# VectorE takes the narrow expert variant first and computes the output places behind the branch; the last MLP outputs go by token part

## The reference

```python
# attention: B=2, H=8, S=576, D=64, causal window of 128, bias by head
attn = softmax(where(mask, q @ k.T / 8 + bias, -1e9));  x = attn @ v      # 1152 tokens x 512

# top-1 MoE: N=1152 tokens, E=8 experts, D=512, F=1024, capacity = N // E * 2 = 288
expert_idx = argmax(x @ w_gate);  gate_w = softmax(x @ w_gate)[expert_idx]
disp[e, slot] = x[i]                      # a token past its expert's capacity is dropped
y = relu(disp @ w1) @ w2;  out[i] = gate_w[i] * y[expert_idx[i], pos[i]]  # 0 if dropped

# MLP: 1152 x 512 -> 2048 -> 512
h = out @ w_in;  result = (h * sigmoid(h)) @ w_out
```

## Time and profile before

| what | us |
|---|---|
| median of 3 runs | 481.11 |
| lowest, highest | 479.75, 485.68 |
| the profiled execution | 479.0 |
| its span, first to last instruction | 477.3 |
| TensorE busy in it | 445.4 (93%) |
| mean granted TensorE clock | 0.975 |

### The profile page before, as it was taken

How to read it: one execution, slowest core, us unless ns; L and a number is a source line. 1 busy time by engine, 2 the same in 40 slices (tenths; PEclk the granted TensorE clock), 3 DMA queues, 4 the chain that set the end, 5 groups by cost and what they waited for, 6 DMA issues and landing times.

```text
span 477.3 us, 8177 instructions
## 1 busy us (share of the span) xinstructions
PE 445.4 (93%) x2917; PEld 406.8 (85%) x2917; DVE 239.7 (50%) x705; ACT 225.7 (47%) x549; POOL 235.5 (49%) x161
## 2 busy tenths in 40 slices
PE   5899989927999999999999999999999999999992
PEld 4677777727999999999999989998999999999982
DVE  4477888874674866857758442122222222222230
ACT  4777768633585656666566644222222222212221
POOL 3006777742879999899898975820200002000002
PEclk9999999956999999999999999999999999999998
DMA  9999940139858777787577600000100000000001
GB/s 182 277 278 291 290 122 12 46 110 320 300 191 276 280 245 227 228 281 274 201 250 253 237 16 1 1 2 0 67 0 0 0 0 32 34 0 0 0 0 66
DMA packets 54566, 64.28 MB, mean 135 GB/s; under 512 B 32096, under 2 KB 32096, under 8 KB 54528
## 3 DMA queue, kind: packets, MB, share of 16 engines
q1 hardware_dynamic: 52752, 59.08, 39.6%
q0 software_dynamic: 1776, 4.73, 2.7%
HBM read 54.35 MB, written 9.44 MB: 134 GB/s over the span
## 4 chain that ended last, share of the span: by engine, by line
PE 84%; DVE 6%; ACT 4%; issue 3%; DMA 1%; POOL 1%; DVEq 0%; POOLq 0%
PE bank L1151 17%; PE bank L1129 14%; PE bank L1130 14%; PE bank L1131 14%; PE bank L1150 8%; PE bank L1003 4%; PE bank L1148 3%; PE bank L1043 3%; PE bank L1020 2%; PE bank L987 2%; PE bank L1149 2%; ACT prob L548 1%; PE bank L1135 1%; DVE prob L724 1%; DVE x_tile L755 1%
## 5 line engine op out<-in xcount | busy, mean ns | idle before, releaser
L439 POOL TENSOR_TENSOR w_lo<-w_raw,w_hi 128x1024 fp32r<-128x1024 f32 x72 | 178.4, 2500 | 39.5 <-ACT w_hi L578 34.8
L959 DVE TENSOR_TENSOR g_full<-bank,sigmoid 128x384 f32<-128x384 f32 x48 | 26.8, 558 | 135.4 <-ACT sigmoid L666 131.6
L666 ACT ACTIVATE sigmoid<-bank 128x384 f32<-128x384 f32 x48 | 23.6, 492 | 132.7 <-PE bank L1131 124.5
L519 POOL DMA_INDIRECT out_dram<-out_stage,permcol x9 | 8.8, 975 | 150.5 <-DVE out_stage L978 148.6
L578 ACT ACTIVATE w_hi<-w_raw 128x1024 fp32r<-128x1024 f32 x74 | 77.7, 1051 | 0.0
L898 DVE TENSOR_REDUCE bank<-bank 128x192 f32<-128x384 f32 x96 | 53.5, 558 | 43.1 <-PE bank L1151 43.0
L1151 PE MATMUL bank<-hidden,w_hi 128*128 128x384 f32 x224 | 67.0, 362 | 0.0
L1129 PE MATMUL bank<-x_hi,w_hi 128*128 x192 | 65.0, 339 | 0.0
L1131 PE MATMUL bank<-x_hi,w_lo 128*128 x192 | 64.6, 336 | 0.0
L1130 PE MATMUL bank<-x_lo,w_hi 128*128 x192 | 64.4, 336 | 0.0
L1151 PE MATMUL bank<-xT,w_hi 128*128 128x384 f32 x192 | 61.2, 366 | 0.0
(11 more groups left out here) (129 smaller groups left out, 792.5 us busy)
## 6 DMA issues: line engine op xcount, KB each, us to landing
w_raw<-in_moe_w_dram SPq DMA_DIRECT2D x64, 512.0 KB, 5.7
dispatch_dram<-zeros SPq DMA_DIRECT2D x4, 1152.0 KB, 7.8
w_raw<-in_moe_w_in_dram SPq DMA_DIRECT2D x8, 512.0 KB, 4.5
w_raw<-in_moe_w_out_dram SPq DMA_DIRECT2D x8, 512.0 KB, 6.7
dispatched<-dispatch_dram SPq DMA_DIRECT2D x9, 384.0 KB, 7.7
q_raw<-in_q_dram SPq DMA_DIRECT2D x8, 256.0 KB, 5.6
k_raw<-in_k_dram SPq DMA_DIRECT2D x8, 256.0 KB, 6.1
v_raw<-in_v_dram SPq DMA_DIRECT2D x8, 256.0 KB, 5.9
```

What stands on the lines that cost most here:

```text
L439: nc.gpsimd.tensor_tensor(wlo[s][:, sl], raw[s][:, sl], whi[s][:, sl], ALU.subtract).then_inc(pool_lo, 1)
L666: nc.scalar.activation(sig[:, f % 2, :], bank[f % 4][:, 0:TB], ACT.Sigmoid).then_inc(sig_ready, 1)
L959: nc.vector.tensor_tensor(gf[:, f % 2, :], bank[f % 4][:, 0:TB], sig[:, f % 2, :], ALU.mult).then_inc(gf_ready, 1)
```

## The change

- VectorE's branch compares the other way round, so that the narrow variant stands first in its code and the wide one behind it. TensorE and ScalarE branch as before.
- The output places are a function that VectorE calls inside the branch, behind the four `x_low` of expert 0. The copy to `permcol` that ended them is gone; `routed` is told by the instruction before it. The wide variant waits for `routed` in addition.
- SyncE does not wait for `routed` any more. GpSimd waits for `offs_ready` ahead of one subtraction and for `routed` ahead of `tell_places`.
- In each MLP block the outputs of the last four chunks (12 to 15) are taken out of the order and done at the end, by token part: all of part 0, then 1, then 2, except that (part 1, chunk 12) comes ahead of (part 0, chunk 15).

```diff
-        def by_top_count(eng, experts):
+        def by_top_count(eng, experts, narrow_first=False):
 
             n = eng.value_load(top[0:1, 0:1], min_val=0, max_val=C)
-            with eng.If(n > NARROW):
-                experts(C)
+            with eng.If(n <= NARROW if narrow_first else n > NARROW):
+                experts(NARROW if narrow_first else C)
             with eng.Else():
-                experts(NARROW)
+                experts(C if narrow_first else NARROW)
...
             load_dispatched(0)
             sp.wait_ge(xd_in, 16)
 
-            sp.wait_ge(routed, 1)
             load_w1(1, 2)
...
+            pool.wait_ge(offs_ready, 2)
             low_here(1, EARLY - PIECES, EARLY + 1)
...
                 low_here(2 + n // PIECES, n % PIECES, split_by(E, 2 * PIECES + n + 1))
+            pool.wait_ge(routed, 1)
             for t in range(NTOK):
                 tell_places(t)
...
-            link(nc.vector.tensor_scalar(pos8[:], pos8[:], -float(C), 0.0, ALU.add, ALU.max))
...
-            link(nc.vector.tensor_copy(target[:], osum[:]))
-            nc.vector.tensor_copy(permcol[:], target[:, 0:TS]).then_inc(routed, 1)
+            def output_places():
+
+                link(nc.vector.tensor_scalar(pos8[:], pos8[:], -float(C), 0.0, ALU.add, ALU.max))
...
+                nc.vector.tensor_copy(target[:], osum[:]).then_inc(routed, 1)
...
+            linked = chain[0]
+
             def experts(w):
+                chain[0] = linked
                 for c in range(KC):
                     dve.wait_ge(step_done, c + 1)
                     dve.wait_ge(hi_ready, c + 1)
                     x_low(c, bank[c], w)
+                output_places()
                 if w > NARROW:
+                    dve.wait_ge(routed, 1)
                     dve.wait_ge(scattered, 16 * NTOK)
...
             dve.wait_ge(offs_ready, 2)
-            by_top_count(dve, experts)
+            by_top_count(dve, experts, narrow_first=True)
...
+            def last_outputs(tb):
+
+                assert TS == 3
+                f0, last_f = F2C - FQ, F2C - 1
+                turns = [(0, f) for f in range(f0, last_f)] + [(1, f0), (0, last_f)]
+                turns += [(1, f) for f in range(f0 + 1, F2C)] + [(2, f) for f in range(f0, F2C)]
+                for t, f in turns:
+                    if t == 0:
+                        pe.wait_ge(glo_ready, tb * F2C + f + 1)
+                    last = output_part(tb, f, t)
+                    if f == last_f:
                         last.then_inc(o_done, 1)
 
             with pe.Fori(0, NB) as tb:
                 for f in range(F2C + 2):
                     if f < F2C:
                         hidden(tb, f)
-                    if f >= 2:
+                    if 2 <= f < F2C - FQ + 2:
                         output(tb, f - 2)
+                last_outputs(tb)
```

More of the change, by code:

```diff
@@ L878, in _ @@
             nc.vector.tensor_copy(offs[:], off8[:]).then_inc(offs_ready, 1)
-            link(nc.vector.tensor_scalar(pos8[:], pos8[:], -float(C), 0.0, ALU.add, ALU.max))
[L881 to L889, removed]
-            link(nc.vector.tensor_copy(target[:], osum[:]))
-            nc.vector.tensor_copy(permcol[:], target[:, 0:TS]).then_inc(routed, 1)
+            def output_places():
+                link(nc.vector.tensor_scalar(pos8[:], pos8[:], -float(C), 0.0, ALU.add, ALU.max))
+                nc.vector.reduce_sum(droprank[:], pos8[:], axis=AX.X)
+                link(nc.vector.tensor_tensor(oo[:], onehot[:], off8[:].unsqueeze(1).broadcast_to([P, NTOK, E]), ALU.mult))
+                link(nc.vector.reduce_sum(osum[:], oo[:], axis=AX.X))
+                link(nc.vector.tensor_tensor(osum[:], osum[:], place[:], ALU.add))
+                link(nc.vector.tensor_scalar(dtot[:], droprank[:], incl8[:, E - 1:E], None, ALU.add))
+                link(nc.vector.tensor_scalar(keep[:], place[:], float(C), None, ALU.is_lt))
+                link(nc.vector.tensor_tensor(osum[:], osum[:], dtot[:], ALU.subtract))
+                link(nc.vector.tensor_tensor(osum[:], osum[:], keep[:], ALU.mult))
+                link(nc.vector.tensor_tensor(osum[:], osum[:], dtot[:], ALU.add))
+                nc.vector.tensor_copy(target[:], osum[:]).then_inc(routed, 1)
             def take_sum(bk, w):
@@ L1214, in hidden, with output_part @@
                 last.then_inc(h2_done, 1)
+            def output_part(tb, f, t):
+                s, fq = f // FQ, f % FQ
+                row = slice(W_IN + fq * DM, W_IN + (fq + 1) * DM)
+                col = slice(t * P, (t + 1) * P)
+                return triple(bank[4 + t][:], ((ghi[:, f % 4, col], glo[:, f % 4, col]), (whi[s][:, row], wlo[s][:, row])),
+                              f == 0, f == F2C - 1)
             def output(tb, f):
-                s, fq = f // FQ, f % FQ
                 pe.wait_ge(glo_ready, tb * F2C + f + 1)
@@ L1222, in output @@
                     pe.wait_ge(o_dve, tb + 1)
-                row = slice(W_IN + fq * DM, W_IN + (fq + 1) * DM)
                 for t in range(TS):
[L1225 to L1228, removed]
+                    output_part(tb, f, t)
+            def last_outputs(tb):
[8 more added lines that the diff above has]
+                    if f == last_f:
                         last.then_inc(o_done, 1)
```

## The result

The change made the kernel slower, by 0.9%: the median is 484.47 us (480.65 to 490.70) against 480.31 us (476.00 to 486.41), ratio 1.009, 95% interval 1.0066 to 1.0113. The forecast was 476.6 us, in a range of 473.5 to 480.5.

The account below looks back on a forecast made before the run. TensorE was taken as the bound (busy 93% of the span), so only its waits could give time. Gains of 3.3 us at the experts' start and 1.2 at the tail took the median from 481.1 to 476.6 us, range 473.5 to 480.5.

Parts of the forecast that it names:

- Start of the experts: Expert stage start: VectorE's branch follows the offsets, so PE's first product comes at 108.1 instead of 111.39; gain 3.3 us.
- The cover of 1.8 us for the branch: Expert start: VectorE ready at 105.7, first `x_high` done at 107.5; a fetch longer than these 1.8 us eats the gain.
- the short bound: Output places behind the fourth `x_low`: 2.5 us for all of them, against 5.2 us as the other bound.
- the delay behind them: Expert 0: VectorE's first sum comes 1.2 us late behind the places; costed at nothing, bounds 0 to 0.8 us.
- The clock at the start: PE's rise to 2.4 GHz in the experts: taken as zero, between 0.7 us gained and 1.7 lost.
- The tail: After the last matmul: the third scatter leaves at 470.4 instead of 471.64; gain 1.2 us.
- The end of DVE's branch: MLP head: VectorE jumps over the wide variant, taken as 4.10 us; cost zero, bounds 0 and 2.6 us.
- 0.35 us were in hand: MLP head: first `g_lo` starts at 274.3, still ahead of 274.66, where POOL's subtraction ends, so PE loses nothing.
- rival (a): MLP head: from 4.5 us of fetch on, `g_lo` misses POOL's gap and 2.6 us are lost; 479.2 us, chance 0.26.
- Rival (d): MLP head: a fetch of some 7 us misses two POOL gaps, 5.3 us lost; 481.9 us, slower than before, chance 0.04.
- The last outputs by token part: End of each MLP block: PE's work the same, group (0, 15) just fits behind its `g_lo`; bound 0.1 us a block.
- a case that needed 0.35 us in hand: Whole kernel: the forecast itself, median 476.6 us, with the jump at the MLP's head costing nothing; chance 0.50.

Follow-up runs that it names:

- VectorE's part: The whole change but with the old `output` and the old order of the MLP outputs; ratio to the kernel before 1.006 (1.0018 to 1.0102).
- order mended: The whole change with output groups (1, 12) ahead of (0, 14) and (1, 13) ahead of (0, 15); ratio to the kernel before 1.0008.
- code shifted: The whole change with 64 never-run memsets added to the wide variant, moving VectorE's code behind it; ratio to the kernel before 0.997.
- branch turned only: The kernel before with only VectorE's branch turned so the narrow variant stands first, places still ahead of it; ratio to before 0.994.

## Why the prediction was wrong

**Start of the experts: right.** Forecast -3.3, measured -3.28 between transposes and product. The cover of 1.8 us for the branch held; in the kernel with only the places moved VectorE's narrow variant again lies behind the wide one, and its start took 1.55 us as well. The places took 2.4 us, the short bound, and the delay behind them cost nothing: PE has no wait in the experts.

**The clock at the start: within the bounds, and the gain was luck.** I put zero, with -0.7 and +1.7 as bounds. It rose at 114.2, 3.0 us behind the first product instead of 4.1: some 0.5 us gained, most of the 0.75 by which the experts were shorter. But among the ten executions whose product followed the transposes by 1.55 us the rise came 2.5 to 5.3 us behind the product. In the two with over 5 us (VectorE's part, order mended) the experts took 156.12 and 156.21 us, longer than before. So the 0.75 us are not an effect of the change.

**The tail: right.** Forecast -1.2, measured -1.27.

**The end of DVE's branch: the step that failed.** The place and the mechanism were named, and it was even said that this part speaks against the change. I took 4.10 us from the branch on entry, cost it at nothing because 0.35 us were in hand, and bounded it at 2.6. It cost 7.7 us (4.84 of wait, 2.85 of clock). Four things in that step were wrong:

- *The size of the fetch.* 4.10 us was no upper bound. At the jump the weights of the last quarter were landing, and the stop took 5.1 to 5.9 us in all kernels with the jump and this load; with the load issued later, 2.8 to 3.0. I had written that these transfers run at the same time, as a point for rival (a), and put no number on it.
- *One fetch or two.* I counted the jump as one stop. The second, 1.75 us, depended on the position of the loop's code. With the code shifted, PE's wait was 2.59 us, 1.5 more than before, and the clock did not fall: without the second stop, less is lost than in rival (a). Nothing in the rows of before could have told its position, but that it may happen should have been a bound.
- *POOL.* I had DVE wait for gaps between POOL's subtractions that run on unmoved. They do not: ACT makes the next `w_hi` behind `g_hi`, which waits for DVE, so POOL ran dry at 273.7 and stood idle for 2.5 us. In two kernels (branch turned only, code shifted) `g_lo` therefore met no subtraction and took 0.56 us. In the change the second stop let POOL start first, and it took 2.02. Rival (d), "slower than before", had the right sign and the right jump, but its mechanism, two missed gaps, did not happen.
- *The clock.* I weighed it at the start only. A wait in which it falls was not priced, and it added more than half of the 4.84 us again. How much it adds varied: the four executions in which it fell during the wait lost 1.95 to 2.85 us by it.

**The last outputs by token part: the second step that failed, and smaller.** I proved that the group (0, 15) just fits and looked at no other. (0, 14) comes as the third group, only 1.4 us behind hidden(15). Its `g_lo` is late because hidden(14) and hidden(15) now follow one another at once: on DVE `g_lo` of chunk 14 stands behind `g_full` of chunk 15. Before, an output lay between the two. Priced at nothing with a bound of 0.1 us a block, it cost 0.41 a block, 1.2 in all, and used up the gain of the tail.

The chances went wrong with it. I gave 0.50 to a case that needed 0.35 us in hand against an unknown of microseconds, and 0.04 to the sign that came.

## What to carry to other kernels

Turning a branch round did not remove its fetch here, it moved it to the end of the variant that stands first: ask what runs at that place, what loads the DMA queues there, and how long the slowest consumer can wait. Work that fits behind a branch was free here, since a transfer covered the branch; take that part and leave the order of the variants alone. And when a new order brings two producers together, check each consumer behind them and not only the last: the queue of the engine between them has changed for all.

## What the hardware showed that I had not expected

- The same jump on VectorE cost 2.79 to 2.97 us with idle DMA engines and 5.1 to 5.9 us while 2 MB of weights were landing (DMA share 0.95). In each case it ended 1.8 to 2.05 us behind an instruction packet; the rest was the time until that packet.
- Where code lies changed a kernel by microseconds: 64 instructions that are never run took the sum from 374.48 to 368.61 us.
- TensorE's clock fell to 1.2 GHz during waits of 5.3 to 5.9 us (for 6.8 to 6.9 us) and 1.4 us behind the end of one of 3.38 us (for 3.41 us). Waits of 1.1 to 2.6 us at the same place left it at 2.4 GHz.
- The pause behind one and the same branch on entry was 4.10 us in one execution and 2.88 us in another. An instruction packet is counted at 108.9 in both, 2.0 us ahead of the pause's end; the DMA share in the pause was 0.82 and 0.52.
